# Moving the low parts of the operands from GpSimd to VectorE ahead of the first block, with V in three uneven parts

## The reference

```python
w = softmax(weight)                                      # (8, 7), per head
x = causal_conv(x, w)                                    # 7 taps along the sequence, per head
h = x.transpose(0, 2, 1) @ U @ V                         # low rank mixing along the sequence
u = x + h.transpose(0, 2, 1)
x = u + maximum(u @ w_ch1, 0) @ w_ch2                    # first layer

X = fft(fft(x, axis=1), axis=2)                          # second layer
u = x + real(X)
un = (u - mean(u)) / sqrt(var(u) + 1e-6)
out = u + maximum(un @ w_ch1b, 0) @ w_ch2b
```

## Time and profile before

| | |
|---|---|
| median of 3 runs | 1306.46 us (1306.34 to 1307.77) |
| the profiled execution | 1305.1 us, its span 1303.1 us |
| PE busy | 1272.1 us, 98% |
| VectorE, ScalarE, GpSimd busy | 781.2, 670.9, 390.1 us |
| mean granted TensorE clock | 0.992 |
| PE convolves pieces 0 and 1 | 10.31 to 17.88 us |
| PE convolves pieces 2 and 3 | from 22.41 (3.65 us), from 27.47 (2.77 us) |
| PE's four groups for t | from 19.79 (9 matmuls, 2.82 us), 25.75 (9, 1.89), 30.27 (9, 1.75), 36.64 (8, 2.31) |
| VectorE's first low of the prologue | 16.35 us |
| first matmul of block 0 | 46.27 us |
| clock 0.50 | 37.2 to 50.8 us |

### The profile page before, as it was taken

How to read it: one execution, slowest core, us unless ns; L and a number is a source line. 1 busy time by engine, 2 the same in 40 slices (tenths; PEclk the granted TensorE clock), 3 DMA queues, 4 the chain that set the end, 5 groups by cost and what they waited for, 6 DMA issues and landing times.

```text
span 1303.1 us, 24636 instructions
## 1 busy us (share of the span) xinstructions
PE 1272.1 (98%) x9064; PEld 1253.0 (96%) x9064; DVE 781.2 (60%) x2041; ACT 670.9 (51%) x1594; POOL 390.1 (30%) x500
## 2 busy tenths in 40 slices
PE   6799999999999999999999999999999999999998
PEld 5699999999999999999999999999999999999998
DVE  4655565666665566555556666655656666665554
ACT  4355555444465555445555555544445555555553
POOL 1322322222233344322222244421101344443331
PEclk9799999999999999999999999999999999999999
DMA  8866642333566532224434222212233222222220
GB/s 284 273 215 209 206 138 92 116 119 114 164 195 211 178 122 71 63 75 135 130 106 144 85 84 84 88 60 86 87 99 102 83 84 88 84 94 82 68 80 29
DMA packets 89023, 157.20 MB, mean 121 GB/s; under 512 B 11128, under 2 KB 44032, under 8 KB 88732
## 3 DMA queue, kind: packets, MB, share of 16 engines
q1 hardware_dynamic: 84872, 149.22, 36.0%
q0 software_dynamic: 4032, 6.41, 1.6%
HBM read 96.68 MB, written 64.47 MB: 124 GB/s over the span
## 4 chain that ended last, share of the span: by engine, by line
PE 95%; DVE 2%; issue 1%; DMA 1%; ACT 0%; POOLq 0%; POOL 0%; DVEq 0%; ACTq 0%
PE bank L693 19%; PE bank L694 9%; PE bank L674 8%; PE bank L682 7%; PE bank L681 7%; PE bank L678 7%; PE bank L675 7%; PE bank L727 4%; PE bank L697 4%; PE bank L775 3%; PE bank L696 2%; PE bank L745 2%; PE bank L744 2%; PE bank L743 2%; PE bank L759 2%
## 5 line engine op out<-in xcount | busy, mean ns | idle before, releaser
L1054 DVE SCALAR_TENSOR_TENSOR ht<-bank,ht 128x384 fp32r<-128x384 f32 x528 | 294.3, 557 | 379.4 <-ACT ht L874 375.3
L874 ACT ACTIVATE ht<-bank 128x384 fp32r<-128x384 f32 x528 | 259.8, 492 | 491.9 <-PE bank L682 489.4
L693 PE MATMUL bank<-w,ht 128*128 128x384 f32 x1320 | 418.3, 366 | 0.2
L694 PE MATMUL bank<-w,ht 128*128 128x192 f32 x1320 | 330.8, 251 | 0.0
L1255 POOL TENSOR_TENSOR ub<-ub,tmp 128x576 f32<-128x576 f32 x88 | 126.1, 1433 | 460.3 <-DVE ub L1062 308.8
L694 PEld LDWEIGHTS bank<-w,ht 128*128 128x128 f32 x1320 | 251.9, 191 | 0.0
L693 PEld LDWEIGHTS bank<-w,ht 128*128 128x128 f32 x1320 | 248.3, 188 | 2.8 <-issue 0.5
L674 PE MATMUL bank<-uth,w1h 128*128 128x384 f32 x528 | 189.0, 358 | 0.1
L682 PE MATMUL bank<-uts,w1t 128*128 128x384 f32 x528 | 179.6, 340 | 0.0
L681 PE MATMUL bank<-uts,w1s 128*128 128x384 f32 x528 | 179.0, 339 | 0.1
L678 PE MATMUL bank<-utl,w1h 128*128 128x384 f32 x528 | 178.8, 339 | 0.0
(11 more groups left out here) (110 smaller groups left out, 2432.7 us busy)
## 6 DMA issues: line engine op xcount, KB each, us to landing
f1t<-f_copy SPq DMA_DIRECT2D x44, 396.0 KB, 3.2
ub<-x_conv SPq DMA_DIRECT2D x44, 288.0 KB, 3.3
x_two<-ub SPq DMA_DIRECT2D x44, 288.0 KB
ub<-x_two SPq DMA_DIRECT2D x44, 288.0 KB, 3.1
mix<-mixed SPq DMA_DIRECT2D x44, 288.0 KB, 3.5
out<-ub SPq DMA_DIRECT2D x44, 288.0 KB
xin<-in_x SPq DMA_DIRECT2D x12, 864.0 KB, 6.2
x_conv<-xin SPq DMA_DIRECT2D x12, 756.0 KB
```

What stands on the lines that cost most here:

```text
L693: e.matmul(dn[t][:, 0:2 * D], hh, w2[ph][:, m, :], start=(m == 0), stop=False)
L694: mm = e.matmul(dn[t][:, 0:D], hl, w2[ph][:, m, 0:D], start=False, stop=False)
L874: e.activation(hth[q % 4], up[q % 3][:, 0:TOK], ACT.Relu).then_inc(act_h, 1)
L1054: e.scalar_tensor_tensor(htl[q % 4], up[q % 3][:, 0:TOK], 0.0, hth[q % 4].bitcast(F32), ALU.max, ALU.subtract).then_inc(dve_l, 1)
```

## The change

- `V_PARTS` is (0, 6), (6, 18), (18, 33) in place of (0, 11), (11, 22), (22, 33). Each part has a buffer of its own (`vpart`); the middle one, `vmid`, lies where zh and zl come later.
- All low parts of the prologue are VectorE's: `u_low(0)`, `u_low(1)`, and `weights_low` in three calls, of which the last (w2) comes in block 0 behind `turned_low(0)`. GpSimd has no tensor work before v_low(1).
- `first_parts` goes through the pairs as 1, 3, 0, 2. ScalarE makes the high parts of a piece before that of U. `sum_t` of the piece before comes ahead of `v_low(0)`.
- ScalarE makes w2's high part in block 0, behind `turned_high(0)`. PE waits for w2's low part ahead of `up_slot(0, 2)`.
- SP issues w2 behind load_v(1) and `mir` behind load_x(1, 0). store_v(1) moves from (0, 5) to (0, 4). load_v(2) moves to (0, 5), and by the condition in `load_v` waits until part 1 is stored.

```diff
-V_PARTS = [(0, 11), (11, 22), (22, N2)]
+V_PARTS = [(0, 6), (6, 18), (18, N2)]
...
+            vmid = early.enter_context(nc.sbuf_tensor("vmid", [4 * R, (V_PARTS[1][1] - V_PARTS[1][0]) * 128], F32R))
...
+        vpart = [ht[0:4 * R, 0:V_PARTS[0][1] * 128], vmid[:], vlate[:]]
...
@@ SP
-            e.dma_start(mir[:], mirror).then_inc(ld_mir, 16)
             load_w1(0, w1a)
             store_x(0, 0)
-            load_w2(0, w2a)
             store_x(0, 1)
             store_x(0, 2)
             store_v(0)
...
             load_v(0)
             load_u(0)
             load_v(1)
+            load_w2(0, w2a)
             load_u(1)
             load_x(1, 0)
+            e.dma_start(mir[:], mirror).then_inc(ld_mir, 16)
             for n in range(4):
                 e.dma_start(vraw[n * R:(n + 1) * R, va:], V[:, va:]).then_inc(ld_v[1], 16)
             copy_f1(0)
             copy_f1(1)
             load_x(1, 1)
-            load_v(2)
...
+                    if (n, m) == (0, 4):
+                        store_v(1)
                     if (n, m) == (0, 5):
-                        store_v(1)
+                        load_v(2)
@@ PE
-            e.wait_ge(w0_l, 1)
-            e.wait_ge(w0_l2, 1)
+            e.wait_ge(w0_l, 2)
             up_slot(0, 0)
             up_slot(0, 1)
...
+                    if (n, m) == (0, 0):
+                        e.wait_ge(w0_l, 3)
@@ ScalarE
+                for k in range(0, PAIRS, 2):
+                    first_high(p, k)
                 if p < len(U_PARTS):
                     u_high(p)
-                for k in range(0, PAIRS, 2):
-                    first_high(p, k)
                 if p == 2:
                     v_high(0)
-            for part in range(3):
-                weights_high(0, part)
+            weights_high(0, 0)
+            weights_high(0, 1)
...
                 if n == 0:
                     turned_high(n)
+                    weights_high(0, 2)
                     hidden(n, 0)
@@ VectorE
+            def u_low(n):
+                a, z = U_PARTS[n]
+                e.wait_ge(u_h, n + 1)
+                e.tensor_tensor(uhl[:, a:z, R:2 * R], u_raw[:, a:z], uhl[:, a:z, 0:R].bitcast(F32), ALU.subtract).then_inc(u_l, 1)
...
             for p in range(NP):
-                for k in range(PAIRS):
+                for k in (1, 3, 0, 2):
                     first_parts(p, k)
+                if p < len(U_PARTS):
+                    u_low(p)
+                if p:
+                    sum_t(0, p - 1)
                 if p == 2:
                     v_low(0)
-                if p:
-                    sum_t(0, p - 1)
-            weights_low()
+            weights_low(0)
             sum_t(0, NP - 1)
             t_low(0)
+            weights_low(1)
...
                     turned_low(n)
+                    weights_low(2)
                     lows(n, 0)
@@ GpSimd
-            for n, (a, z) in enumerate(U_PARTS):
-                e.wait_ge(u_h, n + 1)
-                e.tensor_tensor(uhl[:, a:z, R:2 * R], u_raw[:, a:z], uhl[:, a:z, 0:R].bitcast(F32), ALU.subtract).then_inc(u_l, 1)
-            e.wait_ge(w0_h, 1)
-            e.tensor_tensor(w1t[0][:], w1t_raw[0][:], w1s[0][:].bitcast(F32), ALU.subtract)
-            lo = w2[0][:, :, D:2 * D]
-            e.tensor_tensor(lo, w2_raw[0][:, :, D:2 * D], w2[0][:, :, 0:D].bitcast(F32), ALU.subtract).then_inc(w0_l2, 1)
```

More of the change, by code:

```diff
@@ L189, in program @@
         with ExitStack() as early:
-            vlate = early.enter_context(nc.sbuf_tensor("vlate", [4 * R, (N2 - V_PARTS[0][1]) * 128], F32R))
+            vlate = early.enter_context(nc.sbuf_tensor("vlate", [4 * R, (N2 - V_PARTS[2][0]) * 128], F32R))
         with nc.sbuf_tensor("steep", [128, H, CT], F32) as steep:
@@ L358, in program @@
         (ld_cw, ld_u, ld_id, ld_mir, ld_tab, ld_tabs, cw_ready, eps_set, taps_zero, taps_set,
-         taps_out, steep_in, band_set, u_h, u_l, v_h, v_l, w0_h, w0_l, w0_l2, w1_h, w1_l, cwc,
+         taps_out, steep_in, band_set, u_h, u_l, v_h, v_l, w0_h, w0_l, w1_h, w1_l, cwc,
          act_un, dve_nm, act_tst, dve_tst, pe_cv, act_x, act_xh, dve_xh, dve_xl, pool_xl, dve_ts,
@@ L364, in program @@
             "ld_cw ld_u ld_id ld_mir ld_tab ld_tabs cw_ready eps_set taps_zero taps_set "
-            "taps_out steep_in band_set u_h u_l v_h v_l w0_h w0_l w0_l2 w1_h w1_l cwc "
+            "taps_out steep_in band_set u_h u_l v_h v_l w0_h w0_l w1_h w1_l cwc "
             "act_un dve_nm act_tst dve_tst pe_cv act_x act_xh dve_xh dve_xl pool_xl dve_ts "
@@ L583, in store_v @@
                 e.wait_ge(v_l, n + 1)
-                src = ht[0:4 * R, 0:z * 128] if n == 0 else vlate[:, (a - V_PARTS[1][0]) * 128:(z - V_PARTS[1][0]) * 128]
-                e.dma_start(vst[:, a:z, :].rearrange("r j p -> r (j p)"), src.bitcast(F32)).then_inc(v_stored[n], 16)
+                e.dma_start(vst[:, a:z, :].rearrange("r j p -> r (j p)"), vpart[n].bitcast(F32)).then_inc(v_stored[n], 16)
             def copy_f1(i):
                 e.dma_start(f1d[:, i], f1[:, i]).then_inc(ld_f1[i], 16)
-            e.dma_start(mir[:], mirror).then_inc(ld_mir, 16)
             load_w1(0, w1a)
             store_x(0, 0)
-            load_w2(0, w2a)
             store_x(0, 1)
@@ L901, in spectrum_high @@
                 i = blocks[n][2]
+                if n == 0:
+                    e.wait_ge(v_stored[1], 16)
                 for half, z, m in ((0, zh, 128), (1, zs, 64)):
@@ L977, in weights_high @@
                     e.wait_ge(ld_w1[n], 48)
-                    copy(w1h[n][:], w1l_raw[n][:])
+                    copy(w1h[n][:], w1l_raw[n][:]).then_inc(w_h[n], 1)
                 elif part == 1:
-                    copy(w1s[n][:], w1t_raw[n][:])
+                    copy(w1s[n][:], w1t_raw[n][:]).then_inc(w_h[n], 1)
                 else:
@@ L989, in v_high @@
                 e.wait_ge(ld_v[min(n, 1)], 64)
-                copy(ht[0:4 * R, 0:z] if n == 0 else vlate[:, a - V_PARTS[1][0] * 128:z - V_PARTS[1][0] * 128],
-                     vraw[:, a:z]).then_inc(v_h, 1)
+                copy(vpart[n], vraw[:, a:z]).then_inc(v_h, 1)
             for p in range(NP):
@@ L1187, in v_low, with weights_low @@
                 e.wait_ge(v_h, n + 1)
-                low = ht[2 * R:4 * R, 0:V_PARTS[0][1] * 128]
+                low = vpart[0][2 * R:4 * R]
                 e.tensor_tensor(low, vraw[2 * R:4 * R, 0:V_PARTS[0][1] * 128], low.bitcast(F32), ALU.subtract).then_inc(v_l, 1)
-            def weights_low():
-                e.wait_ge(w0_h, 1)
-                e.tensor_tensor(w1l[0][:], w1l_raw[0][:], w1h[0][:].bitcast(F32), ALU.subtract).then_inc(w0_l, 1)
+            def weights_low(part):
+                e.wait_ge(w0_h, part + 1)
+                low, raw, high = ((w1l[0][:], w1l_raw[0][:], w1h[0][:]), (w1t[0][:], w1t_raw[0][:], w1s[0][:]),
+                                  (w2[0][:, :, D:2 * D], w2_raw[0][:, :, D:2 * D], w2[0][:, :, 0:D]))[part]
+                e.tensor_tensor(low, raw, high.bitcast(F32), ALU.subtract).then_inc(w0_l, 1)
+            def u_low(n):
+                a, z = U_PARTS[n]
+                e.wait_ge(u_h, n + 1)
+                e.tensor_tensor(uhl[:, a:z, R:2 * R], u_raw[:, a:z], uhl[:, a:z, 0:R].bitcast(F32), ALU.subtract).then_inc(u_l, 1)
             e.wait_ge(steep_in, 16)
@@ L1288, in second_low @@
                 if part == 0:
-                    e.wait_ge(w_h[1], 1)
+                    e.wait_ge(w_h[1], 3)
                     e.tensor_tensor(w1l[1][:], w1l_raw[1][:], w1h[1][:].bitcast(F32), ALU.subtract)
@@ L1311, in v_low @@
                 e.wait_ge(v_h, n + 1)
-                low = vlate[2 * R:4 * R, a - V_PARTS[1][0] * 128:z - V_PARTS[1][0] * 128]
+                low = vpart[n][2 * R:4 * R]
                 e.tensor_tensor(low, vraw[2 * R:4 * R, a:z], low.bitcast(F32), ALU.subtract).then_inc(v_l, 1)
```

## The result

The changed kernel takes 1310.28 us (median of 10 runs, 1307.22 to 1313.24), the kernel before 1306.35 (10 runs, 1305.14 to 1307.77). The ratio is 1.0032, with a 95% interval of 1.0022 to 1.0042. The change makes the kernel slower by some 4 us. 1311.4 was forecast. The profiled execution took 1309.5 us (1310.0 was forecast) and has a span of 1307.6 us, 4.5 above the span before.

What follows compares the result with a forecast made beforehand. PE, busy for 98% of the span, was taken to bound the kernel. A third low_rank 3.2 us late plus 1.7 us of clock loss gave +4.9 on the median of 1306.46, so 1311.4 us, range 1309.5 to 1313.

Steps and rivals of the forecast that it cites:

- Prologue: Ahead of block 0: VectorE's lows end earlier, `ub` is added at 37.05 instead of 43.75, block 0 starts 6.7 us earlier.
- w2: Second weights, issued behind load_v(1), land near 42, wanted at 40: some 2 us of wait in block 0, covered.
- Step 1: V's raw remainder lands at 53.2 us, with w2 and `mir` ahead in the queue and larger quarters.
- Steps 2 and 3: After V's landing, ScalarE's v_high(1) takes 1.5 us, to 54.7, then GpSimd's v_low(1) 3.5, to 58.3.
- Step 4: SP's store_v(1) goes out at 58.35 and lands 4.8 us later, at 63.2.
- Step 5: load_v(2) goes at 63.2 and lands in 2.5 us, at 65.75, so the third low_rank is 3.2 us late.
- The clock: Behind PE's gap at the third low_rank the clock drops, losing 1.7 us of work; bounds 0 and 3.5.
- (b): Rival: V's remainder moves at 400 GB/s, lands at 48.0, prologue's gain partly kept, 1303.1 to 1304.5 us; chance 0.13.
- (a): Rival: the same wait at the third low_rank, but the clock holds: +3.2, so 1309.7 us; chance 0.18.
- (c): Rival: w2 and V's larger quarters cost less, V lands at 50 to 52, 1304.5 to 1309 us; chance 0.19.
- (d): Rival: VectorE isn't done sooner, load_u(0) only 2 us earlier in the prologue: +5.2 +1.7, 1313.4 us; chance 0.08.

Runs made afterwards that it cites:

- kernels without waits: Three kernels: the changed one with V cut at 9 and 21 and V's work in later slots, two also with a single V load: 1301.57, 1300.96, 1300.32 us.
- one-DMA run: Changed kernel with V's raw columns loaded by one DMA of 128 partitions instead of four of 32: 1306.41 us, ratio 0.9999 to the kernel before.
- V ahead of x: Changed kernel with V's four raw loads ahead of load_x(1, 0) and `mir` in SP's order: 1310.49 us, ratio 1.0038 to the kernel before.
- cut at 11: Changed kernel with V's old parts (0, 11), (11, 22), (22, 33) and load_v(2) back in the prologue: 1303.80 us, ratio 0.9984 to the kernel before.
- cut at 9: Changed kernel with V's parts (0, 9), (9, 21), (21, 33) and load_v(2) back in the prologue: 1303.89 us, ratio 0.9990 to the kernel before.
- the queue off: First of the kernels without waits, plus V's raw columns in one DMA, with load_v(2) and load_u(2) issued ahead of it: 1300.96 us, ratio 0.9964.

## Why the prediction was right

Direction, size and mechanism held: +4.9 us were forecast, 4.5 came in the span of the profiled execution and 3.9 between the medians. By its steps:

- **Prologue.** Forecast: first group for t at 17.9, load_u(0) at 34.15, `ub` added at 37.05. Measured: 18.88, 33.47, 36.35. Right, with PE's first two pieces slower than counted (they end at 18.69, not at 17.88) and SP's way through the last stores to load_u(0) faster (5.2 us, not 6.0). The forecast priced GpSimd's surplus (5.1 us less on VectorE against 3.5 more) and called the rest order; it did not say what each moves load_u(0) by. The runs give 0.3 to 0.6 us to the engine, 3.2 to the order of the pairs, about 1 to part 0's size (11 for 6).
- **w2.** Forecast to land near 42, it landed at 40.0 and cost ScalarE 0.76 us and PE nothing. Covered it is only while V's wait is there: of the kernels without waits two have PE idle for 0.88 and 0.89 us until w2's low part is made, a price of w2's new place that is still to be won back.
- **Step 1, V's landing.** 53.2 forecast, 53.1 measured, and by the one-DMA run for the reason given: 32 partitions a transfer. (The 223 GB/s that the forecast found to agree with its 218 are 2% above it; the changed kernel has 206.)
- **Steps 2 and 3** (ScalarE 1.5, GpSimd 3.5): 1.49 and 3.47.
- **Step 4**, the store: 4.8 forecast, 4.4 measured. This is the term that was most mis-sized. The queue ahead of it had drained more than I counted (from 58 to 62 us 298 GB/s at a share of 0.74, before the change 380 at 0.95). **Step 5**: 2.5 forecast, 2.35 measured. Together the low_rank came at 65.04 and not 65.8, 2.45 us late and not 3.2. That the total still comes near 4.9 is helped by 0.35 us that no step of the forecast has.
- **The clock.** 1.7 forecast for the second gap, 1.7 measured. That it was due at all is in part luck: behind gaps of 2.2 and 2.5 us at the same place, two of the experiments lost nothing. The first gap's cold stretch (0.57 from 55.5 to 59.5) was absorbed by the second wait.
- **The rivals.** (b), V at the full rate, is what the one-DMA run makes on purpose. It came out at 1306.4, not at 1303.1 to 1304.5. V landed at 47.91 and the low_rank was at 60.06, as its sum said (48.0 and 60.6), but the rival left out that PE then arrives earlier too and that its gap costs the clock. (a) was real in two of the experiments (clock 1.00 behind gaps of 2.2 and 2.5 us) but not here. (c) falls by V's landing at 53.1, (d) by load_u(0) at 33.47.

## What to carry to other kernels

When an early stage gets faster, follow each transfer that its end triggers to its next consumer, and add up that row: here landing, copy, subtraction, store and reload took 27 us from issue and decided the time of block 2's low_rank. A part cut smaller to start sooner moves its work to the next part, so ask who needs the next part first. Where data is replicated over partition groups, load it in one transfer over all partitions rather than one for each group (here it needed the input laid out four times in HBM). Work moved off one wait meets the next: in the last three kernels PE still waited 0.5 to 0.9 us here and there, each time for something that the longer waits had hidden. So read the trace again after each move.

## What the runs showed of the hardware

- While V's rows moved (44 to 48 us), four loads of 32 partitions gave 206 GB/s at a DMA share of 0.94, one of 128 partitions 403 at 0.98.
- A VectorE instruction with two SBUF inputs beside a GpSimd tensor instruction took 3.45 us, against 0.76 alone. By the rows it is held back rather than slower: in the five stretched rows of VectorE (three before the change, 3.44 and 3.45 in the kernels without waits) the instruction ends 0.41 to 0.81 us after GpSimd's, which is its own length alone less 0.13 to 0.15. Those with one input in PSUM weren't touched: in the changed kernel two `ht` instructions of VectorE beside GpSimd's v_low(2) (58.23 to 62.53) took 0.56 us each, as elsewhere.
- PE's gap and the clock behind it aren't one to one. After gaps of 3.0, 4.1 and 6.4 us at the third low_rank the next 10 us ran at 0.83, 0.83 and 0.79, after 2.2 and 2.5 at 1.00. But before the change a gap of 1.9 us was followed by 0.57, and behind ScalarE's wait for V gaps of 2.0 (V ahead of x) and 2.2 us (cut at 11) were followed by 0.59 and 0.70 over 4 us, one of 1.15 (cut at 9) by 1.00. The gap of 1.68 us that all eleven traces share was followed by 1.00 in ten and by 0.57 in one.
- A drop cost the same 1.7 us of work in eight cases: before the change behind the first gap (0.72 over 6.0 us), in the changed kernel behind both gaps (0.74 over 6.5 and 0.83 over 10), with one DMA (0.83 over 10), with the cut at 9 behind a gap of 2.1 us (0.67 over 5.2), with the cut at 11 (0.74 over 6.7), with V ahead of x behind the first gap (0.73 over 6.2), and at 541 us with the queue off (0.57 over 3.9). It cost 2.1 behind the gap of 6.4 us. In the two kernels whose clock held behind the low_rank, the drop before it had cost 2.7 and 2.8 (0.72 over 9.7, 0.70 over 9.4), under the wait for `vch`.
